# A transformer block with two expert layers on one core: the constant rows, two small loads and the gate splits of the attention stage are made in other places

## What is computed

```python
# attention: q, k, v are (2, 8, 576, 64), s is (2, 8, 576)
cum = np.cumsum(np.maximum(s, 0.0), axis=-1)
bias = -(cum[:, :, :, None] - cum[:, :, None, :])
scores = np.where(causal, -1e9, q @ k.T / 8 + np.minimum(bias, 0.0))
attn = softmax(scores);  x = attn @ v            # -> x is (1152, 512)
# first expert layer: 8 experts, each token goes to its best two (noisy logits)
logits = x @ w_gate + log1p(exp(x @ w_noise)) * noise
out[token] += weight * (relu(x @ w1[e]) @ w2[e])
# second expert layer: all 8 experts on all tokens, weights P balanced in 8 rounds
out += P[:, e:e + 1] * (relu(x @ w1[e]) @ w2[e])
```

## Time and profile before

| | |
|---|---|
| runs | 1200.61, 1198.19 and 1200.26 us, median 1200.26 |
| the profiled execution | 1204.84 us |
| its span, first to last instruction | 1203.1 us |
| TensorE busy in the span | 1188.2 us (99%) |
| VectorE, ScalarE, GpSimd busy | 697.3, 426.4, 254.8 us |
| mean granted TensorE clock | 0.993 |

### The profile page before, as it was taken

How to read it: one execution, slowest core, us unless ns; L and a number is a source line. 1 busy time by engine, 2 the same in 40 slices (tenths; PEclk the granted TensorE clock), 3 DMA queues, 4 the chain that set the end, 5 groups by cost and what they waited for, 6 DMA issues and landing times.

```text
span 1203.1 us, 20068 instructions
## 1 busy us (share of the span) xinstructions
PE 1188.2 (99%) x7085; PEld 1062.0 (88%) x7085; DVE 697.3 (58%) x1584; ACT 426.4 (35%) x918; POOL 254.8 (21%) x303
## 2 busy tenths in 40 slices
PE   8999999999999999999999999999999999999998
PEld 6999888888888888889889899899899898898997
DVE  6664775554444451657566575575574675665753
ACT  7675344444344241224123232242241241332320
POOL 8767111111111456201001011011010010110110
PEclk9998999999999999999999999999999999999999
DMA  7770654444455420013120220210211201202102
GB/s 179 182 173 4 246 179 153 155 150 153 180 180 203 161 61 1 1 36 106 36 71 6 64 70 0 70 40 30 70 35 35 70 24 46 70 0 70 35 1 78
DMA packets 40230, 102.81 MB, mean 85 GB/s; under 512 B 4750, under 2 KB 23694, under 8 KB 38010
## 3 DMA queue, kind: packets, MB, share of 16 engines
q1 hardware_dynamic: 33722, 85.70, 22.7%
q0 software_dynamic: 3360, 11.01, 3.0%
q10 hardware_dynamic: 3104, 5.54, 1.4%
HBM read 87.82 MB, written 10.30 MB: 82 GB/s over the span
## 4 chain that ended last, share of the span: by engine, by line
PE 95%; DVE 2%; ACT 1%; DMA 1%; issue 1%; POOL 0%; DVEq 0%; POOLq 0%
PE bank L1164 10%; PE bank L1163 10%; PE bank L1162 9%; PE bank L1118 9%; PE bank L1116 9%; PE bank L1117 9%; PE bank L940 5%; PE bank L942 5%; PE bank L941 5%; PE bank L922 5%; PE bank L924 4%; PE bank L923 4%; PE bank L847 3%; PE bank L828 1%; PE bank L792 1%; PE bank L829 1%
## 5 line engine op out<-in xcount | busy, mean ns | idle before, releaser
L1164 PE MATMUL bank<-part2h,partl 128*128 128x512 f32 x504 | 198.6, 394 | 0.0
L1163 PE MATMUL bank<-part2l,parth 128*128 128x512 f32 x504 | 197.6, 392 | 0.0
L761 POOL TENSOR_TENSOR part2l<-raw_part,part2h 128x512 fp32r<-128x512 f32 x56 | 72.4, 1293 | 589.9 <-ACT part2h L1414 589.9
L1162 PE MATMUL bank<-part2h,parth 128*128 128x512 f32 x504 | 195.7, 388 | 0.0
L1886 DVE SCALAR_TENSOR_TENSOR x_sb<-bank,share_now,x_sb 128x512 f32<-128x512 f32 x126 | 94.1, 747 | 159.5 <-PE bank L1164 159.5
L1118 PE MATMUL bank<-x_forms,forml 128*128 128x288 f32 x448 | 132.1, 295 | 0.0
L1116 PE MATMUL bank<-x_forms,formh 128*128 128x288 f32 x448 | 131.9, 294 | 0.0
L1117 PE MATMUL bank<-x_forms,formh 128*128 128x288 f32 x448 | 131.8, 294 | 0.0
L1565 DVE SCALAR_TENSOR_TENSOR hl<-bank,hh 128x336 fp32r<-128x336 f32 (+1 forms) x88 | 45.7, 519 | 131.5 <-ACT hh L1291 131.3
L922 PE MATMUL bank<-xTh,w1h 128*128 128x336 f32 (+1 forms) x352 | 115.9, 329 | 0.7 <-DVE xTl L1545 0.5
L923 PE MATMUL bank<-xTl,w1h 128*128 128x336 f32 (+1 forms) x352 | 113.9, 324 | 0.0
(11 more groups left out here) (244 smaller groups left out, 2464.2 us busy)
## 6 DMA issues: line engine op xcount, KB each, us to landing
raw<-in_w SPq DMA_DIRECT2D x15, 2048.0 KB, 7.7
raw_part<-in_w1b SPq DMA_DIRECT2D x14, 1024.0 KB, 6.0
raw_part<-in_w2b SPq DMA_DIRECT2D x14, 1024.0 KB, 6.1
k_raw<-in_kT SPq DMA_DIRECT2D x16, 288.0 KB, 5.3
y_dram<-x_sb ACTq DMA_DIRECT2D x16, 256.0 KB, 4.4
q_raw<-in_qT SPq DMA_DIRECT2D x8, 288.0 KB, 5.0
q_two<-w2l SPq DMA_DIRECT2D x8, 288.0 KB, 5.8
x_dram<-x_sb SPq DMA_DIRECT2D x1, 2304.0 KB, 9.2
```

The lines of the kernel that those rows point to most:

```text
L1162: pe.matmul(dst, parth[:, l, ts], part2h[:, l, :], start=(l == 0), stop=False)
L1163: pe.matmul(dst, parth[:, l, ts], part2l[:, l, :], start=False, stop=False)
L1164: mm = pe.matmul(dst, partl[:, l, ts], part2h[:, l, :], start=False, stop=(l == FL - 1))
```

## The change

- The relu of s moves from VectorE to ScalarE, and the small copy into `rinv` from the fill to step -1.
- `second_cum`, twice, moves from SP's queue to ScalarE's, behind the first round of q.
- The constant rows of slot 2 (`k_top[2]` and `q_top[2]`) are no longer written by GpSimd but copied by three DMAs on SP's queue from the constant tiles `ones` and `causal`, behind `double_q(1)` and ahead of `load_raw(2)`. The `q_top` rows of slot 1 move from ScalarE to GpSimd.
- The two small stores of the sums and `load_cum` stay with SP.
- The first warm-up is 5 matmuls of 256 columns instead of 3 of 512, and `keep_warm` has 128 columns in all of the 13 steps.
- The six operations of `split_gates` are spread over the steps 57, 58, 59, 62, 63 and 64.

```diff
-        WARM_UPS = 3
+        WARM_UPS = 5
-        W1_LOW_AT, EARLY_AT, GATES_AT = ALL - 4 * DC, ALL - ST, 60
+        W1_LOW_AT, EARLY_AT, GATES_AT = ALL - 4 * DC, ALL - ST, (57, 58, 59, 62, 63, 64)
-        SECOND_LATER, LAST_ROWS_AT = 2, 4
+        SECOND_LATER = 2
@@ SP @@
             def load_cum(h):
-                if h < HEADS_RING:
-                    sp.wait_ge(aug_ready, 2 + h)
                 if h == 1:
+                    sp.wait_ge(rows_filled, 3)
                     sp.wait_ge(cum_stored, 32)
-            def second_cum(row, part):
-                sp.dma_start(k_top[0][row:row + 1, S:N].bitcast(F32), part[FIRST_ROWS + 1:FIRST_ROWS + 2, :].bitcast(F32)).then_inc(cum_loaded[0], 16)
+            def copy_rows(to, constant, cols):
+                times = N // cols
+                shape = [to.shape[0], times, cols]
+                sp.dma_start(to.rearrange("p (a c) -> p a c", a=times).bitcast(F32),
+                             constant.unsqueeze(1).to_broadcast(shape)).then_inc(rows_copied, 16)
             sp.wait_ge(cum_high, 1)
-            sp.wait_ge(aug_ready, 2)
-            second_cum(HD, cum_h)
             sp.dma_start(cum_rows[:, 0, :], cum_h[CUM_ROWS, :].bitcast(F32)).then_inc(cum_stored, 16)
             sp.wait_ge(cum_low, 1)
-            second_cum(HD + 1, cum_l)
             sp.dma_start(cum_rows[:, 1, :], cum_l[CUM_ROWS, :].bitcast(F32)).then_inc(cum_stored, 16)
...
             double_q(1)
+            copy_rows(k_top[2][HD + 2:P, :], ones[HD + 2:P, :], P)
+            copy_rows(q_top[2][HD + 2:P, :], causal[HD + 2:P, 0:3 * P], 3 * P)
+            copy_rows(q_top[2][HD:HD + 2, :], ones[HD:HD + 2, :], P)
             sp.wait_ge(low, LOWS)
             load_raw(2)
@@ GpSimd @@
-            for w in range(HEADS_RING):
-                pool.memset(k_top[w][HD:P, :].bitcast(F32), 1.0).then_inc(aug_ready, 1)
-            pool.memset(q_top[2][HD:P, :].bitcast(F32), 0.0).then_inc(q_rows_clear, 1)
+            for w in range(2):
+                pool.memset(k_top[w][HD:P, :].bitcast(F32), 1.0).then_inc(rows_filled, 1)
+            pool.memset(q_top[1][HD:P, :].bitcast(F32), 0.0).then_inc(rows_filled, 1)
+            pool.wait_ge(rows_filled, 4)
+            pool.wait_ge(q_rows_ready, 1)
+            pool.memset(q_top[1][HD:HD + 2, :].bitcast(F32), 1.0).then_inc(q_rows_ready, 1)
...
-                if k == LAST_ROWS_AT:
-                    pool.wait_ge(q_rows_clear, 1)
-                    pool.wait_ge(q_rows_ready, 2)
-                    pool.memset(q_top[2][HD:HD + 2, :].bitcast(F32), 1.0).then_inc(q_rows_ready, 1)
@@ TensorE @@
-                    if h < HEADS_RING:
+                    if h < 2:
                         pe.wait_ge(q_rows_ready, h + 1)
+                    if h == 2:
+                        pe.wait_ge(rows_copied, 48)
...
-                keep_warm(BANK)
+                keep_warm(BANK // 2)
...
-                    keep_warm(BANK // 2 if k < -SCORES_AHEAD else P)
+                    keep_warm(P)
@@ ScalarE @@
+            act.wait_ge(s_loaded, 32)
+            act.activation(cum_p[0:CUM_END, :], cum_s[0:CUM_END, :], ACT.Relu, scale=SQRT_D).then_inc(s_positive, 1)
             act.wait_ge(const_ready, 6)
             act.wait_ge(first_rows, 1)
-            for w in range(2):
-                act.activation(q_top[w][HD:P, 0:S], causal[HD:P, 0:S], ACT.Relu, bias=row_ones[HD:P, 0:1], scale=0.0)
-                act.activation(q_top[w][HD:P, S:N], causal[HD:P, 0:S], ACT.Relu, bias=row_ones[HD:P, 0:1], scale=0.0).then_inc(q_rows_ready, 1)
+            act.activation(q_top[0][HD:P, 0:S], causal[HD:P, 0:S], ACT.Relu, bias=row_ones[HD:P, 0:1], scale=0.0)
+            act.activation(q_top[0][HD:P, S:N], causal[HD:P, 0:S], ACT.Relu, bias=row_ones[HD:P, 0:1], scale=0.0).then_inc(q_rows_ready, 1)
...
             act.copy(q_top[0][0:HD, 0:S], q_raw[:, 0, 0:S]).then_inc(first_high, 1)
+            act.wait_ge(rows_filled, 2)
+            act.wait_ge(cum_high, 1)
+            second_cum(HD, cum_h)
+            act.wait_ge(cum_low, 1)
+            second_cum(HD + 1, cum_l)
             act.wait_ge(k_again[0], 16)
@@ VectorE @@
-            link(v.tensor_copy(rinv[:].rearrange("p a b -> p (a b)"), ones[:, 0:2 * STEPS]))
-            v.wait_ge(s_loaded, 32)
-            link(v.tensor_scalar(cum_p[0:CUM_END, :], cum_s[0:CUM_END, :], 0.0, SQRT_D, ALU.max, ALU.mult))
+            v.wait_ge(s_positive, 1)
...
-                if k == GATES_AT:
-                    split_gates()
+                if k == -1:
+                    link(v.tensor_copy(rinv[:].rearrange("p a b -> p (a b)"), ones[:, 0:2 * STEPS]))
+                if k in GATES_AT:
+                    split_gates(GATES_AT.index(k))
```

More of the change, by code:

```diff
@@ L204, in build @@
         s_loaded = sem("s_loaded")
+        s_positive = sem("s_positive")
+        rows_copied = sem("rows_copied")
         cum_summed = sem("cum_summed")
@@ L210, in build @@
         ident_rounded = sem("ident_rounded")
-        q_rows_clear = sem("q_rows_clear")
         q_rows_ready = sem("q_rows_ready")
@@ L224, in build @@
         const_ready = sem("const_ready")
-        aug_ready = sem("aug_ready")
+        rows_filled = sem("rows_filled")
         rough_ready = sem("rough_ready")
@@ L597, in _ @@
             pool.memset(causal[:], 0.0).then_inc(const_ready, 1)
-            pool.memset(aug[:].bitcast(F32), 0.0).then_inc(aug_ready, 1)
+            pool.memset(aug[:].bitcast(F32), 0.0).then_inc(rows_filled, 1)
             pool.memset(v_sb[:, :, :, 0:1], 1.0).then_inc(const_ready, 1)
@@ L1202, in place_max, with second_cum @@
                 act.copy(q_top[w][ROWS_ROUGH:ROWS_ROUGH + 2, b * S + i0:b * S + i1], bank[0:2, MAX_AT, 0:i1 - i0]).then_inc(max_placed, 1)
+            def second_cum(row, part):
+                act.dma_start(k_top[0][row:row + 1, S:N].bitcast(F32), part[FIRST_ROWS + 1:FIRST_ROWS + 2, :].bitcast(F32)).then_inc(cum_loaded[0], 16)
             def high_k(h, half):
@@ L1459, in _ @@
             v.wait_ge(cum_high, 1)
-            v.wait_ge(aug_ready, 2)
+            v.wait_ge(rows_filled, 2)
             v.scalar_tensor_tensor(out=k_top[0][HD:HD + 2, 0:S], in0=cum_h[0:2, :].bitcast(F32), scalar=row_sign[0:2, 0:1],
@@ L1516, in token_low, with split_gates @@
                                 xTh[:, :, ts].bitcast(F32), ALU.subtract).then_inc(st.xTl_ready, 1)
[L1518 to L1521, removed]
+            def split_gates(step):
+                which, part = divmod(step, 3)
+                cn, c0, g0 = ((2 * E, 0, 0), (E, 2 * E, 4 * E))[which]
+                high, low = gate_w[:, :, g0:g0 + cn], gate_w[:, :, g0 + cn:g0 + 2 * cn]
+                if step == 0:
+                    v.wait_ge(gates_loaded, 48)
+                if part == 0:
                     link(v.tensor_copy(high, gates[:, :, c0:c0 + cn]))
+                elif part == 1:
                     link(v.tensor_tensor(low, gates[:, :, c0:c0 + cn], high.bitcast(F32), ALU.subtract))
+                else:
                     link(v.tensor_tensor(fold[which][:], ident[0:2 * cn, 0:cn], ident[0:2 * cn, cn:2 * cn], ALU.add))
-                assert count[0] == GATES_SPLIT, count[0]
+                assert step < 5 or count[0] == GATES_SPLIT, count[0]
             for k in range(-ROUGH_AHEAD, ALL):
@@ L1908, in _ @@
             far_half(E - 2, 1, False)
-GATES_SPLIT = 5 + 6
+GATES_SPLIT = 4 + 6
 def kernel(q, k, v, s, moe_w_gate, moe_w_noise, moe_noise, moe_w1, moe_w2, moe2_w_gate, moe2_w1, moe2_w2):
```

## The result

The changed kernel takes **1217.01 us** in the median of 4 runs (1215.86 to 1218.22), against 1200.43 of the kernel before on the same chip (4 runs, 1198.19 to 1200.71): ratio 1.0142 [1.0124, 1.0160]. So it is slower, as forecast, but by 16.6 us and not by 8.7, and 1.0 us above the top of the range.

A forecast was written before the change was run, and what follows sets the result against it. TensorE was taken as the bound. From the profiled 1204.84 us, +9.0 copies, +3.0 clock, -1.1 and -4.3 gates gave 1211.4; the median forecast was 1209.0 us, midway between 1206.9 and 1211.2, range 1199.0 to 1216.0.

The forecast's parts named there:

- What bounds the kernel, and where the change acts: TensorE, busy 1188.2 of 1203.1 us, is the bound; the change touches the fill and a low-clock stretch at 90 to 120 us.
- The first tile: Start of the fill: first rough tile at 7.6 instead of 9.10 us, 1.5 earlier, counted as 0 at the end.
- The three copies: SP's queue ahead of head 2's loads: two of sixteen engines carry them, head 2's k lands late, +9.0 us.
- The clock in the fill: TensorE, some 8 us nearly idle before head 2, drops to the lower clock: +3.0 us.
- The gates: Spreading the six gate operations removes a 1.1 us stall and 4.3 us of low clock: -5.4 us against the profiled execution.
- two branches: Timed runs have the gates' clock fall, median 1206.9 us, or do not, 1211.2; the middle, 1209.0, was taken.
- (a): Copies spread over all engines, clock holds in the fill, gates' stall gone: about 1197.5 us, chance 0.14.
- (b): As (a), but TensorE waits 2.2 us in the fill and its clock falls: 3.0 on top, 1200.5 us, chance 0.09.
- (c): Copies on two engines at the slow rate, k of head 2 15.9 us later: 1215.9 us, chance 0.12.
- Copies landing 10 us or more after issue: Sign in the profile: the two large copies on SP's queue land at least 10 us after they go out.
- The clock at 0.5 between 25 and 45: Sign in the fill: the PEclk row shows 0.5 somewhere between 25 and 45 us.
- The first tile of head 2 at about 37: Sign on TensorE: head 2's first tile runs at about 37 us, instead of 27.84.

## Why the prediction was wrong in size

**What bounds the kernel, and where the change acts: right.** TensorE stayed at 98 to 99% busy, and all but 0.9 us of the difference was found where it ran dry or had the lower clock, in the fill and at the gates.

**The first tile: right in time, its worth right for a reason not seen.** 7.6 was forecast and 7.60 measured. But the sixth rough tile ran at 13.29 instead of 12.65, behind a wait of 2.36 us, and the clock was 0.50 from 14.5 to 21.3 us. In the changed kernel the wait for head 2 covers it, as the term of 0 has it. Without the copies the first mark is 1.8 us later than before, so "the same wait covers it" was right of this kernel and could not be counted on in a repaired one.

**The three copies: the mechanism right, the term mis-sized. This is the step that failed.** It said that k of head 2 lands 9.0 us later and the first tile with it; ScalarE's copy of k came 13.14 us later and the tile 13.75 (27.84 to 41.59). The two large copies ran on two of sixteen engines, as taken. The failed choice is the rate: "12 us, near the faster rate, since little else is being moved then". I took two engines' part of the fastest stretch of 426 GB/s, but the two moved 35 to 40 GB/s with nothing else on DMA, near the slow end of 32. Both copies and the two engines' part of the three loads are 0.57 + 0.11 MB; at 35 to 40 GB/s that is 17.0 to 19.4 us, where my 12 plus 2.3 made 14.3. The difference, 2.7 to 5.1 us, takes in the 4.1 by which k was later than I said. The other 0.6 us arose between ScalarE's copy of k and the tile: 5.63 us instead of 5.02, and 5.21 in the kernel with matmuls in both waits, where the clock is 1.00, so some 0.4 of it go with the clock. That the other fourteen engines stood idle did not make these two faster. The sum is rough. For the kernel with one copy it gives 0.40 MB, 9.9 to 11.4 us, and k at 27.4 to 28.9 with the prediction's start at 16.5 and its 1 us to the semaphore, for which no run here has a row; k landed there at 29.85 (issued at 21.75, 8.1 us). From 22 to 28 us all sixteen engines are busy in that kernel and move 209 to 234 GB/s, of which two engines' part would be 26 to 29 (an estimate by equal shares). So in company the two may be slower than the 35 to 40 that they show alone.

The Trainium skill's rule, in "DMA: Bandwidth & Descriptors", section "Why a DMA increments its semaphore by 16 and not by 1", gives 62 rows two engines, and with 48 and 14 rows sixteen and fourteen. The trace agrees: shares of 0.13 to 0.14 and of 0.92.

That SP itself would be held wasn't in the prediction. It put the loads into their queues 8 us later. By the sum above, in which the two engines are busy until k lands, that adds little for these loads; this is argued, no run separates it, and the 1 to 2.5 us that the sum lacks with one copy may be its part. What the hold does delay is whatever else SP has to issue, as `double_k` in the kernel with the copies behind the loads.

**The clock in the fill: +3.0, measured +4.8.** The stretch from the first tile of head 2 to the second mark took 20.44 us instead of 15.63, and 15.55 with the clock held. I had discounted the row at the gates, 4.3 us, for a fall that ends while TensorE still waits. It didn't end: the clock was 0.50 from 31.5 us, in the wait, to 52.0.

**The gates: -5.4, measured -5.35, or -6.0 to step 79.** No operation of TensorE between the marks at 98.73 and 121.99 waits, the clock is 1.00 there, and VectorE has idle time left behind three of the six operations (0.62, 0.51 and 0.40 us).

**The sum and the median.** Against the profiled execution: 13.75 + 4.8 - 5.35 = 13.2, measured 13.38. That it fits so well is partly luck: with the 6.0 it is 12.5, which is what step 79 shows, and 0.9 us came later in code that is the same. For the median I had two branches and took their middle. The runs lie near the second: 1200.26 + 13.75 + 4.8 - 1.1 = 1217.7, or 1216.2 with the 2.6 us that the gates alone gained by the ratio in place of the 1.1; measured 1217.01. The clocks of the timed runs say the same, at most 15 of 75 with the whole fall. The middle was a hedge between two cases and stood for neither. Of the 8.0 us that the forecast was short, some 4.7 are the copies, 1.8 the clock in the fill, and the rest the middle between the branches.

**The rivals.** (a) and (b), copies over all engines, didn't happen; the cut into 48 and 14 rows is their picture, and its 1.0013 is near the "same" of (b). (c), the slow rate, was nearest with 1215.9, and had 0.12. Its nearness is in part luck: its 15.9 us for k was 2.8 too much and its 3.0 for the clock 1.8 too little. For it I had named the pieces of 128 columns; they are not the cause of the two engines. Whether longer pieces would make an engine faster wasn't tried.

**The signs.** Copies landing 10 us or more after issue: the profile gives no landing for transfers of 62 rows, but 0.57 MB at 35 to 40 GB/s takes 14 to 16 us. DMA well under 100 GB/s, a wait of 8 to 11 us on ScalarE (10.84), ten steps of 12 us at the gates (12.00 to step 59 and 11.26 to step 69, where three rough tiles are missing) and a clock of 1.00 there: seen. The clock at 0.5 between 25 and 45: seen, but it lasted to 52. The first tile of head 2 at about 37: 41.59.

## What to carry to other kernels

Ask of every DMA how many engines it gets before asking how many bytes it moves: a block of 62 rows ran on two, the same block as 48 and 14 rows took DMA's share from 0.13 to 0.92. Price such a transfer by the bytes of its few engines at the slowest rate per engine that the trace shows, and add to them the part of every later transfer that falls to the same engines. Constants that an idle engine can write (0.9982 with GpSimd's memsets, 1.0013 with the cut copies) don't belong ahead of a load that gates the pipeline; and where one stall ends in a fall of the clock, count the clock in full: here it was a quarter of the 18.6 us lost in the fill.

## What the runs showed that I had not expected

- SP's issue of the DMA behind a copy of 62 rows took 6.38, 6.48 and 7.04 us, and the same 6.38 when that DMA was a load of 64 rows. Behind the copies of 48 and 14 rows the issues took 0.72 to 1.61. That SP waits until the two engines have caught up is my reading; no run shows what it waits for.
- TensorE's clock fell after short waits amid busy work (2.36, 2.22 and 2.00 us in the fill, 1.09 at the gates of the kernel before), but not after 1.43 in another kernel: the length of the wait alone doesn't sort them. TensorE could then be busy at the 0.50 level for 3.4 us (14.4 to 17.9, small loads by SP) up to 31 (42.3 to 73.7, copies behind the loads) before 1.00 came back. In the changed kernel it was 14.8 us, 8 of them without a pause in

```profile
42.00:50.00 8.00, 8.00 (x36) 7.57 (x35) 2.02 (x6) 1.78 (x4) 6.19 (x12) 0.50 0.44 93
```

- The two stores of the sums, 36 KB each, took 3.5 and 2.5 us to land before and 5.9 and 5.1 after the change, issued some 2.5 us earlier; why is open. Putting the small loads of the sums on a queue of their own didn't make the tile that needs them earlier (12.83 and 12.88).
